# Attention and routed experts on one core: the first load split, constants moved, early routing hops moved

## The reference

```python
scores = scale * np.matmul(q, k.transpose(0, 1, 3, 2))
kth = np.partition(scores, -top_k, axis=-1)[..., -top_k:-top_k + 1]
attn = softmax(np.where(scores >= kth, scores, -1e9))
x = np.matmul(attn, v)                        # then heads side by side: (4, 576, 512)
...
fresh_e = int(np.argmax(logits[b, s]))
if s == 0 or local_gate[b, s] < 0.5:
    e = fresh_e
else:
    e = prev_e
h = np.maximum(x[b, s] @ w1[e], 0.0)
out[b, s] = p[e] * (h @ w2[e])
```

## Time and profile before

| | us |
|---|---|
| median of 3 runs (lowest to highest) | 1013.66 (1013.32 to 1015.21) |
| the profiled execution, its own time | 1011.88 |
| its span | 1010.0 |
| VectorE busy | 762.0 (75%) |
| TensorE busy | 791.0 (78%) |
| GpSimd busy | 613.7 (61%) |
| ScalarE busy | 419.4 (42%) |

### The profile page before, as it was taken

One profiled execution on the slowest core, in us unless ns is written; L12 is line 12 of the kernel. 1 busy time (PEld: TensorE's weight loads), 2 busy tenths in 40 slices (PEclk: granted clock), 3 DMA queues, 4 the chain that ended last, 5 costly groups with the idle time before them and its releaser, 6 DMA issues.

```text
span 1010.0 us, 16010 instructions
## 1 busy us (share of the span) xinstructions
PE 791.0 (78%) x3938; PEld 445.9 (44%) x3939; DVE 762.0 (75%) x1624; ACT 419.4 (42%) x914; POOL 613.7 (61%) x557
## 2 busy tenths in 40 slices
PE   2566666766766766567998889878888999999996
PEld 1343433434433443354554545545454444444442
DVE  5999999999999999899999999999944111111110
ACT  2445555544545555434565565656540111111111
POOL 0878887787878788568888888888812111101111
PEclk7667686676667577657999999999989999999998
DMA  3081001010101104010146145254135155454500
GB/s 122 1 352 65 20 31 49 2 48 13 36 13 35 48 0 142 1 48 22 60 178 235 55 183 219 81 205 184 57 146 188 51 190 208 189 195 162 232 22 27
DMA packets 17498, 103.98 MB, mean 103 GB/s; under 512 B 2638, under 2 KB 5198, under 8 KB 13328
## 3 DMA queue, kind: packets, MB, share of 16 engines
q1 hardware_dynamic: 10560, 57.68, 15.3%
q10 hardware_dynamic: 3024, 34.21, 8.6%
q0 software_dynamic: 3840, 11.28, 3.2%
HBM read 93.72 MB, written 10.75 MB: 103 GB/s over the span
## 4 chain that ended last, share of the span: by engine, by line
DVE 35%; PE 29%; issue 27%; POOL 3%; ACT 2%; DVEq 2%; DMA 1%; ACTq 0%; POOLq 0%
DVE top L978 19%; DVE work L986 13%; PE ps L681 10%; PE ps L686 10%; POOL p_sb L1277 2%; DVEq L200 2%; PE ps L522 1%; PE ps L403 1%; PE ps L670 1%; PE ps L432 1%; PE ps L514 1%; DMA wg_sb<-in_wg 1%; POOL p_sb L1280 1%; PE ps L662 1%; ACT p_sb L767 1%
## 5 line engine op out<-in xcount | busy, mean ns | idle before, releaser
L1277 POOL TENSOR_SCALAR p_sb<-s_sb,top 128x576 f32<-128x576 f32 x141 | 314.5, 2231 | 92.4 <-DVE top L978 89.2
L978 DVE MAX8 top<-work 128x8 f32<-128x576 f32 x432 | 302.4, 775 | 0.0
L403 PE MATMUL ps<-id_sb,p_sb 128*128 128x128 f32 x720 | 134.6, 331 | 184.6 <-ACT p_sb L767 184.6
L1280 POOL TENSOR_TENSOR p_sb<-p_sb,s_sb 128x576 f32<-128x576 f32 x141 | 198.6, 1409 | 26.2 <-POOL p_sb L1277 25.4
L986 DVE MATCH_REPLACE8 work<-top,work 128x576 f32<-128x576 f32 x288 | 213.8, 773 | 0.0
L403 PEld LDWEIGHTS ps<-id_sb,p_sb 128*128 128x128 f32 x720 | 99.0, 169 | 231.5 <-issue 231.5
L1174 DVE TENSOR_SCALAR moe<-ps 128x512 f32<-128x512 f32 x30 | 20.8, 692 | 193.3 <-PE ps L681 193.3
L393 PE MATMUL ps<-qk_sb 64*128 64x288 f32 (+1 forms) x640 | 140.5, 578 | 6.8 <-DMA qk_sb<-in_qk 5.9
L775 ACT ACTIVATE pT_sb<-ps 128x640 f32<-128x640 f32 x144 | 101.4, 704 | 104.7 <-PE ps L403 102.2
L767 ACT ACTIVATE p_sb<-p_sb,nmax 128x576 f32<-128x576 f32 x144 | 110.9, 770 | 79.4 <-POOL p_sb L1280 78.5
L432 PE MATMUL ps<-pT_sb,v_sb 128*64 128x64 f32 (+5 forms) x1152 | 123.5, 378 | 8.7 <-ACT pT_sb L775 8.7
(11 more groups left out here) (155 smaller groups left out, 678.2 us busy)
## 6 DMA issues: line engine op xcount, KB each, us to landing
w_sb<-in_w SPq DMA_DIRECT2D x16, 2048.0 KB, 12.6
w_sb<-in_w ACTq DMA_DIRECT2D x16, 2048.0 KB, 10.6
qk_sb<-in_qk SPq DMA_DIRECT2D x16, 864.0 KB, 4.6
v_sb<-in_v SPq DMA_DIRECT2D x16, 320.0 KB, 2.9
x_dram<-x_sb SPq DMA_DIRECT2D x2, 1024.0 KB, 5.8
x_dram<-x_sb SPq DMA_DIRECT2D x2, 768.0 KB, 4.6
x_dram<-x_sb SPq DMA_DIRECT2D x2, 256.0 KB, 2.4
wg_sb<-in_wg ACTq DMA_DIRECT2D x1, 292.0 KB, 8.1
```

Of the source, the lines that this page charges most:

```text
L403: mm = pe.transpose(ps[:, bank + c // 4, (c % 4) * P:(c % 4 + 1) * P], p_at(n % GROUP)[:, c * P:(c + 1) * P], id_sb[:, :])
L978: dve.max(top[:, par, j, rnd, :], src).then_inc(chain, 1)
L1277: pool.tensor_scalar(p_at(j)[:, 0:S], s_at(n % RING), top[:, k % 2, j, ROUNDS - 1, 7:8], -BIG, ALU.is_lt, ALU.mult).then_inc(masked, 1)
L1280: pool.tensor_tensor(p_at(j)[:, 0:S], p_at(j)[:, 0:S], s_at(n % RING), ALU.add).then_inc(added, 1)
```

## The change

Four things change.

- The load of Q and K of the first unit is issued in two halves, the first batch's and the second's, with a semaphore of its own for the first (`qk_first`). No waits stand before them. SyncE's queue then takes, in this order: Q and K of the second unit, the identity, V of both units, the gate's weights, the small constants, the candidates, the token numbers. ScalarE issues none of them any more.
- VectorE waits for the constants and casts two of them behind round 0 rather than before it. GpSimd waits for the token numbers only where it uses them, after the last round.
- The hops of the early routing move: on TensorE the count's sum from (2, 1) to (2, 0), the turning of the places from (3, 0) to (2, 1), the product of the marks from (3, 1) to (3, 0); on VectorE the placing from (3, 2) to (3, 0), the marks from (4, 0) to (3, 2), the row numbers from (4, 3) to (4, 1).
- GpSimd makes the first two gathers in step 3 rather than 4 and has its wait for the row numbers there. The list of slots for the experts' parts begins one slot earlier and has 38 entries rather than 37, so 15 of 29 parts come one slot earlier.

```diff
         def early_parts():
-            at = [(q, j) for q in range(FROM, STEPS - 1) for j in range(SLOTS)][1:]
+            at = [(q, j) for q in range(FROM, STEPS - 1) for j in range(SLOTS)]
...
-            load_units(0)
+            for t in range(2):
+                part = slice(t * (S + HALF), (t + 1) * (S + HALF))
+                sp.dma_start(qk_sb[:, 0, t, :], qk[0][:, part]).then_inc(qk_in[0] if t else qk_first, 16)
+            sp.dma_start(qk_sb[:, 1, :, :].rearrange("p t s -> p (t s)"), qk[1]).then_inc(qk_in[1], 16)
+            sp.dma_start(id_sb[:, :], ident).then_inc(consts_in, 16)
+            for a in range(2):
+                sp.dma_start(v_sb[:, a, :, :, :].rearrange("p t c d -> p (t c d)"), v[a]).then_inc(v_in[a], 16)
+            sp.dma_start(wg_sb[:, :], wg).then_inc(consts_in, 16)
+            sp.dma_start(small_sb[:, :], small).then_inc(consts_in, 16)
+            sp.dma_start(cand_sb[:, :], cand).then_inc(consts_in, 16)
+            sp.dma_start(tok_sb[:, :, :].rearrange("p n c -> p (n c)"), tokid).then_inc(tok_in, 16)
...
                 t = 2 * TPU * r + n
-                if i == 0:
+                first = isinstance(r, int) and r == 0 and a == 0
+                if first and i == 0:
+                    pe.wait_ge(qk_first, 16)
+                if i == (FULL if first else 0):
                     hold(pe, qk_in[a], 16 * (r + 1))
...
-                elif (k, j) == (2, 1):
+                elif (k, j) == (2, 0):
                     count = early_rows[0]
                     pe.wait_ge(early_counted, 1)
...
-                elif (k, j) == (3, 0):
+                elif (k, j) == (2, 1):
                     row = early_rows[2]
                     pe.wait_ge(early_placed, 1)
...
-                elif (k, j) == (3, 1):
+                elif (k, j) == (3, 0):
                     pe.wait_ge(early_marked, 2)
...
         def _(act):
-            act.dma_start(tok_sb[:, :, :].rearrange("p n c -> p (n c)"), tokid).then_inc(tok_in, 16)
-            act.dma_start(id_sb[:, :], ident).then_inc(consts_in, 16)
-            act.dma_start(small_sb[:, :], small).then_inc(consts_in, 16)
-            act.dma_start(cand_sb[:, :], cand).then_inc(consts_in, 16)
-            act.dma_start(wg_sb[:, :], wg).then_inc(consts_in, 16)
...
-            dve.wait_ge(consts_in, 64)
-            dve.tensor_copy(idb_sb[:, :], id_sb[:, :]).then_inc(idb_ready, 1)
-            dve.tensor_copy(lanes[:, :], lane_row)
...
-                elif (k, rnd) == (3, 2):
+                elif (k, rnd) == (3, 0):
                     dve.wait_ge(early_base_ps, 1)
...
-                elif (k, rnd) == (4, 0):
+                elif (k, rnd) == (3, 2):
                     dve.wait_ge(early_placed, 1)
...
-                elif (k, rnd) == (4, ROUNDS - 1):
+                elif (k, rnd) == (4, 1):
                     dve.wait_ge(early_rows_ps, 1)
...
             largest(0, True)
+            dve.wait_ge(consts_in, 64)
+            dve.tensor_copy(idb_sb[:, :], id_sb[:, :]).then_inc(idb_ready, 1)
+            dve.tensor_copy(lanes[:, :], lane_row)
...
             def early_moves(q):
-                if q == FROM:
+                if q == FROM - 1:
                     pool.wait_ge(early_row_in, 1)
                     pool.wait_ge(x_out, 16 * B)
                     early_gather(0)
...
-            pool.wait_ge(tok_in, 16)
             biases(0, 0)
...
             pool.wait_ge(tiled, 1)
+            pool.wait_ge(tok_in, 16)
```

More of the change, by code:

```diff
@@ L206, in build @@
         qk_in = [sem(f"qk_in{a}") for a in range(2)]
+        qk_first = sem("qk_first")
         v_in = [sem(f"v_in{a}") for a in range(2)]
```

## The result

The changed kernel takes 1018.62 us (median of 16 runs, 1014.65 to 1024.48); the kernel before, run beside it on the same chip, 1015.27 us (16 runs, 1011.09 to 1017.70). The ratio is 1.0037, with an interval of 1.0023 to 1.0050: **slower by about 0.4%**, some 3.7 us. I had forecast 1014.3 us and no change that can be told. Of the 4.3 us between 1014.3 and 1018.62, 1.6 are the starting point: I had added my +0.7 us to 1013.66 us, the median of three runs, and the kernel before came out at 1015.27 us in sixteen. What the change itself adds is 3.7 us by the ratio, where I had 0.7. The profiled execution of the changed kernel took 1016.72 us (span 1014.9, granted clock 0.843), that of before 1011.88.

What follows compares the result with a forecast made beforehand. VectorE's instruction stream was taken to bound the kernel until about 731 us. Start -4.3, hops 0, gathers +5.0 and experts' parts 0 gave +0.7 us on 1013.66: 1014.3 us, no change that can be told, range 1010.0 to 1017.0 us.

Steps and rivals of the forecast that it cites:

- Part one, the start: Kernel start: first matmul at 3.95 us and match_replace at about 9.0 rather than 13.54 us; gain 4.3 us.
- Rival B: At the start, the first half shares DMA engines and lands at 5.87 us: net +2.6 us, 1016.3 us; chance 0.14.
- Part two, the hops: Early routing, groups 3 and 4: the same work moves within VectorE's stream, TensorE's moves are covered; no gain or cost.
- Part three, the gathers: Step 3: GpSimd stands still 4.6 us for the row numbers, VectorE idles 5.3 us before group 5; loss 5.0 us.
- the second stall: At the group after group 5: scores at 470.7 us, VectorE busy until 472.4 us, so no second stall.
- the last 0.29 us: VectorE's 0.29 us wait for a copied score tile at 467.35 us, claimed to go away without gathers in step 4.
- Rival A: At the early gathers, VectorE doesn't feel them: only the gains are left, -4.6 us, 1009.1 us; chance 0.18.
- The sum up to group 6: From the start to group 6: gain 4.3 us and loss 5.0 us, together +0.7 us.
- The experts' parts: Behind the early gathers: not on VectorE, and the last of them keep their slots (20 to 22); cost 0.
- Rival C: Steps 4 to 9: VectorE waits at one or two more groups, 1 to 1.5 us each; +3 us, 1016.7 us; chance 0.10.
- GpSimd's slack: After group 5: GpSimd needs some 12 us for a group of 14.5 us; held against a longer stall.
- What comes after 731 us: Kernel's end: it keeps its shape and moves with VectorE's end, 0.5 to 1 us later than before.

Runs made afterwards that it cites:

- e7: e1 with the first unit's Q and K in one whole load rather than halves; one run, read by its start alone: first matmul at 5.74 us.
- e1: The kernel before with the change's start alone (halved load, constants in SyncE's queue, late casts): 1011.05 us against 1014.57, ratio 0.9984.
- e3: The changed kernel with the old slots and the first two gathers back in step 4, leaving start and hops: 1012.59 us against 1014.57, ratio 1.0002.
- e9: The changed kernel with the old slots, the exponent of e6 and the gathers of e5: 1007.18 us, ratio 0.9915 to the kernel before.
- e6: e1 with ScalarE's exponent of the early logits in slot (1, 1) rather than (2, 0): 1007.26 us against 1014.75, ratio 0.9922.
- e5: The changed kernel with step 3's wait and two gathers behind the third mask rather than the first: 1015.47 us against 1014.75, ratio 0.9998.
- e2: The changed kernel with the old list of 37 slots; start, hops and gathers as changed: 1015.51 us against 1014.57, ratio 1.0027.
- e4: The kernel before with the new list of 38 slots alone, the first part kept at its old slot: 1020.5 us, ratio 1.0066.
- e8: The changed kernel with the scatters of tiles 0 and 2 one step later, so steps 7 and 12 have a gather alone: 1017.23 us, ratio 1.0022.
- e12: The changed kernel, new slots kept, with every early gather and scatter behind the third mask of its step: 1010.36 us against 1014.98, ratio 0.9959.
- e10: e9 with every early gather and scatter behind the third mask of its group: 1003.04 us against 1014.52, ratio 0.9879.

## Why the prediction was right and where it failed

**Part one, the start: right where it is made, wrong at the end.** Gain 4.3 us forecast; 4.33 us measured to the `match_replace`, less the casts' 0.27 us: 4.1 us. First matmul at 4.19 us (forecast 3.95), first `match_replace` at 9.21 us (9.0). The two load rows of the kernel before gave the half 3.25 us, and it took 4.19 - 0.75 = 3.4 us. Rival B falls. (Its first load shared with eight others, not seven.) The Trainium skill (DMA: Bandwidth & Descriptors, section Issuing engines are not separate DMA queues) has loads on the shared 16 engines interleave, from which I had taken that the first half would land with the whole; the trace disagrees to this extent, that the half was in at 4.19 us and the whole of e7 at 5.74 us. The fit of the Trainium skill that the prediction used (DMA: Bandwidth & Descriptors, section Anatomy of one DMA) is given there for DMAs that GpSimd issues, and these loads are SyncE's: the estimate from it, 3.0 us for the half, compares with 3.4 us measured.

What failed is the use of this gain in the sum. It stands there as -4.3 us off the whole time. With nothing else changed the runs have 1.6 us of it (e1, at most 3.4 by the interval), and with the hops none (e3, 1.0002, at most 1.4). The profile of e1 shows where it goes, into waits of VectorE behind group 7.

**Part two, the hops: right.** e9 beside e6 shows no cost. No gap stands at the moved places, and group 3 still ends where the sum had it: in the changed kernel the marks run at 428.68 us, behind the third pass of group 3, and group 4 starts at 433.06 us, where the sum has 437.50 - 4.3 = 433.2.

**Part three, the gathers: right in mechanism and about right in size.** In the ratio of the runs their cost is 4.0 us by e5 and 2.5 us between e3 and e2, where the sum has 5.0. In the profile GpSimd's idle time is 5.20 us against 4.6, VectorE's 4.79 against 5.3 (from the row numbers at 441.87 us to the next mask at 444.57 us are 2.70 us, not the 3.11 of the earlier trace rows, since 0.6 us of idle time ahead of the first issue fell into the wait), the second stall absent, the last 0.29 us gone. The path ran as written, through turn, scores and copy, and not through the masks. TensorE was at 1.2 GHz on it (turn of 1.30 us at 449.48 us), as I had taken. Rival A, that VectorE doesn't feel the gathers, falls; in e5, with the gathers two masks later, it is what happens.

**The sum up to group 6** was +0.7 us and came to +0.07 in the profiled execution.

**The step that failed** is the last one of the sum: that behind group 6 nothing more happens to VectorE ("From there to the end all of it should lie 0.5 to 1 us later than before"). It rests on "until then the time is the length of VectorE's instruction stream" and on "The experts' parts are not on VectorE ... 0". Engines that aren't VectorE set when its score tiles come, and the cover there is thin: the waits for score tiles behind group 6, put at nothing, came to 3.89 us in the changed kernel's profile. In the runs it shows twice.

- *The gain of the start, taken as -4.3 us off the whole.* The runs have -1.6 us (e1) or +0.2 us (e3). By the runs this is the larger part: e3 is 4.5 us above what the sum has for start and hops, and in this chain of kernels the gathers then cost 2.5 us less than the sum has (e2 beside e3) and the list 1.0 us more (the changed kernel beside e2), together 3.0 us. Each of these figures has about 1.6 us of uncertainty to either side or more, so the split is a hint; that the start's gain is not there in full is outside the intervals of e1 and e3.
- *The experts' parts, taken as 0.* The step looked at the last parts, which keep their slots, and took the 15 that move one slot earlier for free. It should have laid out GpSimd's list for each step: with the old list steps 7 and 12 have one transfer each between the first and the second mask, with the new one they have two, 3.0 us of GpSimd from the small sums to the next mask. The earlier trace rows had the price of two, 3.11 us, and the earlier trace rows showed that it reaches VectorE. The forecast used that price for the gathers, gave step 7 half a microsecond in its upper bound, and left step 12 out. In the profiles this costs 3.5 us up to the last group (718.67 to 722.20 us), of which the gaps of groups 14 to 16 are shown to come from the list (e4) with the pair in step 12 (e8, but for 0.54 us at group 16) and the transfers' place (e12). In the runs the list is worth 1.0 us between e2 and the changed kernel and nothing between e3 and e5, both within the intervals; put into the kernel before it costs 6.7 us, with a gap of 4.55 us that the changed kernel doesn't have.

Rival C named the mechanism, with about the right size (1 to 1.5 us at one or two groups; measured 0.51 to 1.49 us at four), and I gave it 0.10 because of "GpSimd's slack". That slack is a sum over the group; what counts is the time from one mask to the next. C was right for step 12 (e8 and e12), not for step 7 (e8), where the gap has a cause that I haven't found.

**The last 1.3 us.** "What comes after 731 us keeps its shape and moves with VectorE's end" was off too. In the changed kernel the last group's start is 3.53 us late, the last part of TensorE ahead of the final turns 728.47 - 723.36 = 5.11 us late, and the logits follow TensorE. The difference arises in one stretch shortly ahead of the last group: TensorE's turn there is 3.80 us late (708.69 to 704.89 us), the expert's part behind it 5.11 us (714.02 to 708.91 us). Windows of 7 us at this place, first of the kernel before, then of the changed one:

```profile
702.89:709.89 7.00, 5.15 (x56) 3.55 (x53) 6.52 (x14) 5.17 (x14) 6.28 (x8) 1.00 0.24 99
```

```profile
706.69:713.69 7.00, 5.00 (x46) 3.26 (x47) 7.00 (x14) 3.31 (x9) 6.28 (x8) 0.76 0.08 29
```

The turn, the scores and the V product there take 1.11, 1.33 and 2.61 us at a granted clock of 0.76 where the kernel before has 0.74, 0.76 and 1.97 us at 1.00, behind 2.35 us of idle TensorE rather than 1.65. It does not hang on the list of slots alone: from the last group to the logits are 29.2 us in before and 28.7 in e2, both at a granted clock of 1.00 from 12 to 5 us ahead of the last group, but 29.5 to 30.3 us in e1, e3, e6, e9 and e10, which have the old list too and 0.74 to 0.87 there, and 29.6 to 30.7 with the new one. What brings the lower clock in some executions I haven't tested.

Both misses together are 4.8 us in the profiled executions; the ratio of the runs has 3.7 us of loss, 3.0 above the forecast. That +0.07 us at group 6 met the +0.7 us of the sum is one execution, and no test of the start's gain over the whole kernel.

## What to carry to other kernels

Edits on engines that aren't the bound are not free when the bound engine waits for what they hand on: write out, step by step, what stands between two consecutive hand-overs, and don't net it over a group. Short fixed costs in an in-order queue, such as the issue of an indirect transfer, belong behind the last hand-over of the group; moving them there from between the first and the second was worth 8 us to the changed kernel (e12), half of it by the first two gathers alone (e5). A gain early in a kernel is not yet a gain of the whole: it counts when the engines that feed the bound one can follow, which the start alone did not get (e1) and, with the transfers out of the way, e10 did. And before a start is optimized it pays to list every wait of the bound engine: the one for the logits' exponent, which the change left alone, was worth 5.1 us, more than the whole start (e6).

## What the runs showed of the hardware that I had not expected

- **Two lengths of the same tail.** Behind the last logits the work is identical, yet it takes 262 us or 264 to 265 us, by whether the granted clock of one stretch of 8 us and the next is 1.00 or about 0.8. It may be a part of the scatter of every kernel here (for the kernel before, 1011.09 to 1017.70 us), but only the profiled executions show it. What decides it I don't know.
- **A small load issued behind large ones is late from either queue.** The candidates, 4 KB, took 6.3 us from issue to landing in the changed kernel, behind the large loads of SyncE's queue, where the halves of Q and K, 432 KB each and issued first, took 3.6 us. In the kernel before they came from ScalarE's queue, where 345 KB in three loads were ahead of them, and took 8.1 us; the token numbers, 27 KB and issued first of all, took 2.4 us. So it is not the order in one queue alone. The DMA issues of the changed kernel over its first 14 us, then one of the kernel before:

```profile
qk_sb<-in_qk SPq DMA_DIRECT2D x2, 432.0 KB, 3.6
...
cand_sb<-in_cand SPq DMA_DIRECT2D x1, 4.0 KB, 6.3
```

```profile
cand_sb<-in_cand ACTq DMA_DIRECT2D x1, 4.0 KB, 8.1
```

- **VectorE and GpSimd slow each other.** The first 64 x 576 scan took 2.13 us in the kernel before, beside an addition and a mask of GpSimd, and that mask took 3.25 us where the others take 2.22. In e6 the scan fell beside GpSimd's small operations; it took 1.45 us, and one of them that elsewhere takes 0.23 us took 1.16:

```profile
406.79 1.45 DVE L1052 TENSOR_TENSOR_SCAN moe<-moe 64x576 f32<-64x576 f32 x1
```

```profile
407.12 1.16 POOL L1225 TENSOR_SCALAR psum_eps<-psum 128x3 f32<-128x3 f32 x1
```
